# Table reads moved into the branches that use them, SyncE's three steps of a tile reordered, and a 64-byte shift of SBUF, in an attention and mixture-of-experts kernel

## The reference

```python
def _attn_ref(x, state):              # x [8,8,512,64], state [8,8,32,64]
    a = softmax(scale * x @ state.T);  xread = a @ state
    a2 = softmax(scale * state @ x.T); sread = a2 @ x
    return concatenate([xread, sread], axis=2)     # 4352 tokens of 512 columns

def _moe_ref(x, w_in, w_out):         # w_in [512,2048], w_out [2048,512]
    h = x @ w_in
    return (h * clip(h + 3, 0, 6) / 6) @ w_out

def _moe2_ref(x, w_gate, w_output_gate, w1, w2):   # 8 experts, w1 [8,512,1024], w2 [8,1024,512]
    e_idx = argmax(x @ w_gate, axis=1)             # each token goes to one expert
    for e in range(8):
        mask = e_idx == e
        out[mask] = gate_w[mask] * eom[mask, e] * (relu(x[mask] @ w1[e]) @ w2[e])
```

## Time and profile before

| | |
|---|---|
| three runs | 1202.80, 1205.89, 1206.66 us; median 1205.89 |
| profiled execution | 1207.43 us, of which the span, first to last instruction, is 1205.7 |
| TensorE | busy 1142.7 us (95%) |
| weight load | 893.1 us (74%), beside the matmuls |
| VectorE | busy 636.8 us (53%) |
| ScalarE | busy 463.8 us (38%) |
| GpSimd | busy 76.9 us (6%) |
| granted TensorE clock, mean | 0.975 of full |
| DMA | 131.65 MB, mean 109 GB/s |

### The profile page before, as it was taken

One profiled execution on the slowest core, in us unless ns is written; L12 is line 12 of the kernel. 1 busy time (PEld: TensorE's weight loads), 2 busy tenths in 40 slices (PEclk: granted clock), 3 DMA queues, 4 the chain that ended last, 5 costly groups with the idle time before them and its releaser, 6 DMA issues.

```text
span 1205.7 us, 21805 instructions
## 1 busy us (share of the span) xinstructions
PE 1142.7 (95%) x6358; PEld 893.1 (74%) x6359; DVE 636.8 (53%) x1247; ACT 463.8 (38%) x780; POOL 76.9 (6%) x96
## 2 busy tenths in 40 slices
PE   9999999999999999999999978889989999869996
PEld 7777777777777777777779866667868888657784
DVE  6675564646546456456644382554453444545543
ACT  4454443444344434444443422443332223333321
POOL 0000101001001010010100110000000000000001
PEclk9999999999999999999999989998989999979999
DMA  9111011101011010000200945747474544746442
GB/s 368 72 36 35 36 36 71 36 1 71 36 35 53 19 71 35 36 36 1 88 18 2 320 144 170 227 158 253 125 261 141 158 145 124 256 138 194 138 146 78
DMA packets 98819, 131.65 MB, mean 109 GB/s; under 512 B 13967, under 2 KB 75023, under 8 KB 94352
## 3 DMA queue, kind: packets, MB, share of 16 engines
q1 hardware_dynamic: 91360, 89.35, 23.4%
q10 hardware_dynamic: 1584, 23.07, 5.1%
q0 software_dynamic: 5760, 17.90, 4.1%
HBM read 85.86 MB, written 45.47 MB: 109 GB/s over the span
## 4 chain that ended last, share of the span: by engine, by line
PE 74%; ACTq 6%; issue 5%; DVE 5%; DMA 3%; ACT 3%; SPq 1%; DVEq 1%; POOL 0%; POOLq 0%
PE y_ps L853 32%; PE h_ps L835 15%; PE y_ps L926 9%; ACTq L442 5%; PE y_ps L910 5%; PE h_ps L910 5%; PE a_ps L810 2%; PE h_ps L825 2%; DMA hid_mv<-hidden 2%; DMA hidden<-expert_hid 1%; ACT we L1074 1%; DVE we L481 1%; DVE act_raw L1551 1%; ACT act_t_hi L1111 1%; PE a_ps L713 1%
## 5 line engine op out<-in xcount | busy, mean ns | idle before, releaser
L853 PE MATMUL y_ps<-w_out_hi,hid_hi 128*128 128x512 f32 x544 | 218.8, 402 | 0.0
L853 PE MATMUL y_ps<-w_out_hi,hid_lo 128*128 128x512 f32 x544 | 212.6, 391 | 0.0
L853 PE MATMUL y_ps<-w_out_lo,hid_hi 128*128 128x512 f32 x544 | 212.3, 390 | 0.0
L926 PE MATMUL y_ps<-we,act_t_hi 128*128 (+1 forms) x608 | 189.1, 392 | 5.4 <-DVE act_t_lo L1558 4.3
L835 PE MATMUL h_ps<-att_hi,mix 128*128 128x512 f32 x512 | 185.3, 405 | 0.1
L1364 DVE SCALAR_TENSOR_TENSOR hid<-hid,h_ps 128x512 f32<-128x512 f32 (+1 forms) x144 | 94.4, 655 | 169.9 <-ACT hid L1033 169.9
L1033 ACT ACTIVATE hid<-h_ps,three 128x512 f32<-128x512 f32 (+1 forms) x144 | 95.3, 662 | 179.1 <-PE h_ps L835 155.5
L853 PEld LDWEIGHTS y_ps<-w_out_hi,hid_hi 128*128 128x128 f32 x544 | 102.1, 188 | 50.6 <-issue 30.4
L926 PEld LDWEIGHTS y_ps<-we,act_t_hi 128*128 128x128 f32 x608 | 114.8, 189 | 31.2 <-issue 6.2
L1373 DVE TENSOR_TENSOR hid_lo<-hid,hid_hi 128x512 fp32r<-128x512 f32 (+1 forms) x144 | 94.8, 658 | 70.4 <-ACT hid_hi L1041 69.9
L910 PE MATMUL h_ps<-we,xg_t_hi 128*128 (+1 forms) x304 | 102.8, 421 | 28.3 <-DVE we L481 14.4
(11 more groups left out here) (216 smaller groups left out, 1457.7 us busy)
## 6 DMA issues: line engine op xcount, KB each, us to landing
raw<-in_w ACTq DMA_DIRECT2D x11, 2048.0 KB, 8.9
hidden<-expert_hid SPq DMA_DIRECT2D x76, 256.0 KB
hid_mv<-hidden SPq DMA_DIRECT2D x152, 128.0 KB, 2.9
xg<-buckets SPq DMA_DIRECT2D x164, 64.0 KB
xb<-in_x_rows SPq DMA_DIRECT2D x8, 1024.0 KB, 4.8
x_t<-in_x_t SPq DMA_DIRECT2D x7, 1024.0 KB, 4.8
buckets<-pad_row SPq DMA_DIRECT2D x8, 774.0 KB, 8.6
raw<-in_w SPq DMA_DIRECT2D x3, 2048.0 KB, 7.7
```

The costliest lines, as they stand in the source:

```text
L853: i = pe.matmul(y_ps[:, t, :], (hid_hi, hid_lo)[hp][:, hid_at(b, j), t * P:(t + 1) * P], w_out_s[wp][:, j, :], start=(j == 0 and m == 0), ...
L926: i = pe.matmul(y2_ps[:, slot % 2, :], act_t[hp][:, slot % 2, f, :], we[:, bass.ds(w_at + (wp * WPART + KD * F + f * DM), DM)], start=(f = ...
```

## The change

Five things are done.

1. ACT reads the two SPLIT numbers ahead of its wait for `hid2_ps`, and everything else inside the branches that use it. In a tile that neither splits nor loads it reads two numbers, not nine.
2. ACT loads the raw `w2` in the same branch and the same tile as the raw `w1`, behind the four pieces of its split of `w2`. It waits there for `w2_ready` of the expert just split, which DVE gives at the end of its own four pieces. Before, this load came one tile later.
3. DVE reads its two SPLIT numbers ahead of `turn_hidden`; before, one behind `hidden_lo` and one at the end.
4. SP writes the hidden values first, then loads rows and gates, then reads back.
5. `rows` takes 8320 bytes instead of 8256, so that all behind it moves by 64 bytes.

```diff
-    o += CH * ROW * 4
+    ROWS_SIZE = -(-CH * ROW * 4 // P) * P
+    o += ROWS_SIZE
...
-    raw1_at = 163840 + CH * ROW * 4 + 2048
+    raw1_at = 163840 + ROWS_SIZE + 2048
...
         def body(t):                                   # SP
-            if not (isinstance(t.n, int) and t.n + 3 >= MT):
-                load_rows(t.plus(3))
-            load_gate(t)
             place = t.slot % 2
...
                 sp.dma_start(hidden[place, :, h * BANK:h * BANK + BANK], expert_hid[:, h * BANK:h * BANK + BANK]
                              ).then_inc(sem("hid_written"), 16)
+            if not (isinstance(t.n, int) and t.n + 3 >= MT):
+                load_rows(t.plus(3))
+            load_gate(t)
             wait(sp, "hid_written", 16 * HALVES * (t.n + 1))
...
                 rows_hi(t.plus(1))                     # ACT
+            split1 = entry(act, t, T_SPLIT)
+            if not t.first:
+                split2 = entry(act, t.plus(-1), T_SPLIT)
             for h in range(HALVES):
                 wait(act, "hid2_ps", HALVES * t.n + h + 1)
...
-            if not (t.first or is_b(t.n, 1)):
-                before_it = t.plus(-2)
-                load = entry(act, before_it, T_LOAD)
-                with act.If(load > 0):
-                    load_w2(entry(act, before_it, T_NEXT, E - 1), entry(act, before_it, T_ORD, E - 3) + 2)
-            if not t.first:
-                before_it = t.plus(-1)
-                load = entry(act, before_it, T_LOAD)
-                with act.If(load > 0):
-                    load_w1(entry(act, before_it, T_NEXT, E - 1), entry(act, before_it, T_ORD, E - 3) + 2)
-                split = entry(act, before_it, T_SPLIT)
-                n = entry(act, before_it, T_ORD, E - 1) + 1
-                other = entry(act, before_it, T_OTHER, WSLOT)
-                first_tile = entry(act, before_it, T_FIRST, MT)
-                with act.If(split > 0):
+                with act.If(split2 > 0):
+                    n = entry(act, before_it, T_ORD, E - 1) + 1
+                    other = entry(act, before_it, T_OTHER, WSLOT)
+                    first_tile = entry(act, before_it, T_FIRST, MT)
+                    load = entry(act, before_it, T_LOAD)
+                    e = entry(act, before_it, T_NEXT, E - 1)
+                    with act.If(load > 0):
+                        load_w1(e, n + 1)
...
                     split_hi(1, n, other)
-            split = entry(act, t, T_SPLIT)
-            n = entry(act, t, T_ORD, E - 1) + 1
-            other = entry(act, t, T_OTHER, WSLOT)
-            with act.If(split > 0):
+                    with act.If(load > 0):
+                        load_w2(e, n + 1)
+            with act.If(split1 > 0):
+                n = entry(act, t, T_ORD, E - 1) + 1
+                other = entry(act, t, T_OTHER, WSLOT)
                 wait(act, "hid2_ps", HALVES * t.n)
                 split_hi(0, n, other)
```

More of the change, by code:

```diff
@@ L1138, in body @@
                 hidden_hi(t.plus(-1))
-            if is_b(t.n, 1):
-                load_w2(entry(act, Tile(0, MT), T_NEXT, E - 1), 1)
-            if not (t.first or is_b(t.n, 1)):
-                before_it = t.plus(-2)
-                load = entry(act, before_it, T_LOAD)
-                with act.If(load > 0):
-                    load_w2(entry(act, before_it, T_NEXT, E - 1), entry(act, before_it, T_ORD, E - 3) + 2)
-            if not t.first:
-                before_it = t.plus(-1)
-                load = entry(act, before_it, T_LOAD)
-                with act.If(load > 0):
-                    load_w1(entry(act, before_it, T_NEXT, E - 1), entry(act, before_it, T_ORD, E - 3) + 2)
-                split = entry(act, before_it, T_SPLIT)
-                n = entry(act, before_it, T_ORD, E - 1) + 1
-                other = entry(act, before_it, T_OTHER, WSLOT)
-                first_tile = entry(act, before_it, T_FIRST, MT)
-                with act.If(split > 0):
+                if is_b(t.n, 1):
+                    load_w2(entry(act, Tile(0, MT), T_NEXT, E - 1), 1)
+                before_it = t.plus(-1)
+                with act.If(split2 > 0):
[6 more added lines that the diff above has]
+                        load_w1(e, n + 1)
                     if not is_b(t.n, 1):
@@ L1568, in body @@
                 put_out(t.plus(-3))
+            split1 = entry(dve, t, T_SPLIT)
             if not t.first:
+                split2 = entry(dve, t.plus(-1), T_SPLIT)
                 turn_hidden(t.plus(-1))
@@ L1575, in body @@
                 before_it = t.plus(-1)
-                split = entry(dve, before_it, T_SPLIT)
-                with dve.If(split > 0):
+                with dve.If(split2 > 0):
                     split_lo(dve, 1, entry(dve, before_it, T_ORD, E - 1) + 1, entry(dve, before_it, T_OTHER, WSLOT),
                              signal="w2_ready")
-            split = entry(dve, t, T_SPLIT)
-            with dve.If(split > 0):
+            with dve.If(split1 > 0):
                 split_lo(dve, 0, entry(dve, t, T_ORD, E - 1) + 1, entry(dve, t, T_OTHER, WSLOT), signal="w1_ready")
```

## The result

| | before | after |
|---|---|---|
| median | 1205.41 us (4 runs) | 1170.62 us (1167.76 to 1174.89, 4 runs) |
| ratio | | 0.9717 [0.9677, 0.9757] |
| profiled execution, its span | 1207.43, 1205.7 us | 1167.76, 1166.0 us |
| TensorE busy | 1142.7 us | 1127.7 us |
| mean granted clock | 0.975 | 0.988 |

1170.6 us were measured where 1171 was forecast. The ratio of 0.9717 makes the gain 34 us, the difference of the medians 34.8. So the trace after shows some 3 us less loss than a usual run has, and a term that comes out better by that much in it is no finding.

What follows compares the result with a forecast made beforehand. ACT's table reads, which leave it behind TensorE at changes of experts, were taken to cause most stage-two losses. 1207.4 - 29.6 (waits and clock) - 4.9 (alignment) = 1172.9, or 1171.4 from the median: forecast 1171, range 1156 to 1187.

Steps and rivals of the forecast that it cites:

- The 9.9 us: ACT's round in a plain tile before the change, table reads included, 1.1 us less than TensorE's.
- first(1): First TensorE block of tile 1: 3.1 us of wait and 2.8 of clock hang on DVE's table building and stay.
- second(1), second(3), first(4), first(5): TensorE blocks of early tiles: tile 1's 4.3 us wait goes; waits of 5.5, 0.4 and 2.1 us remain, plus 2.5 clock.
- pairs at 7, 12, 25, 28, ahead of second(T): Tiles where two raw loads follow closely: the late readback delays TensorE's second block, 1.8 us each, 7 us in all.
- first(28): TensorE's first block of tile 28: late hidden values delay its weight split, 6.9 us of wait and 1.8 of clock remain.
- second(37), the end: Last tile's second block: today's 1.1 us wait stays and SP's order adds 1.1 us, 2.2 in all.
- alignment: Moving SBUF data by 64 bytes makes each tile's first TensorE block 0.13 us faster, 4.9 us in all; bounds +1 and -10.
- one block from E + 6.3 to E + 18.5: Both raw loads' packets flow unbroken, counted from E, the end of tile T's first TensorE block; readback through at E + 20.5.
- rival 1: Raw loads and SP's transfers don't collide, or whole packets hold: the pairs cost 0, 22 us lost or less, 1159; chance 0.20.
- the rule of whole packets: Queues: 9 to 17 descriptors a turn, so the readback passes within the first raw load; the sum 7 us better.
- SP's order is hidden in plain tiles: Plain tiles: readback at most 1.5 us later, landing at E + 10.4, hidden by 8.7 us.
- rival 2: Pairs of raw loads cost 5 us each, first(28) 14, and waits above 2 us bring half clock: 1189; chance 0.20.

Runs made afterwards that it cites:

- e2: The kernel before with only ACT's table reads changed, the second weight load still one tile later: 1181.76 us, 0.9787.
- e6: The kernel before with ACT's raw weight loads cut to a sixteenth, so that they don't hold up SP's transfers: 1197.52 us, 0.9913.
- e7: The changed kernel with ACT's raw weight loads cut to a sixteenth: 1159.61 us, 0.9601.
- e1: The kernel before with only the 64-byte shift of what lies behind `rows` in SBUF: 1204.77 us, 0.9978.
- e5: The kernel before with only SP's new order of writes, loads and readback: 1213.31 us, 1.0045.

## Why the prediction was right

**What bounded the kernel: right.** Nine reads made ACT's round nearly as long as TensorE's 11.07 us, and each change of experts left it behind. The 9.9 us that I worked out are rough: the row that they rest on ends in a wait for TensorE. Rounds without one take 9.4 us (copies of rows at 932.83 and 942.20), and one with a turn of the loop 12.5 (910.40 and 922.88), by the pause that I had nowhere. The mean over four tiles is 10.2, which leaves 0.9 us to spare and not 1.1. e2 takes only reads and gains 25.7 us; e6 takes only the transfers away, and the waits for rows stay. The plain tile came out as worked out: no idle time behind `act_t_hi`, and two reads that lie within the 8.3 us in which ScalarE waits for TensorE anyway.

**The ledger**, place by place, waits and clock in the profiled execution:

| place | forecast | measured |
|---|---|---|
| first(1) | 5.9 | 3.3 + 1.8 |
| second(1), second(3), first(4), first(5) | 8.0 + 2.5 clock | 0.3 + 1.5 + 0.8 + 3.0, clock in the rest |
| pairs at 7, 12, 25, 28, ahead of second(T) | 7 | 0 |
| first(9), by ACT | 0 | 2.1 |
| first(28) | 8.7 | 7.6 + 1.9 |
| second(37), the end | 2.2 | 2.6 |
| clock elsewhere, tiles 1 to 5 too | | 1.9 |
| sum | 34.3 | 26.8 |
| alignment | -4.9 | -1.7 ahead of stage two, -0.8 in it |

The sum of the savings, 34.5 us, met the medians' 34.8 by luck, because two terms that failed offset each other: the alignment brought 2.5 where I had 4.9, and the ledger then 34.8 - 2.5 = 32.3 where I had 29.6.

**The step "one block from E + 6.3 to E + 18.5" failed.** The two raw loads are 6.6 us apart as forecast (856.51 and 863.12 at tile 12), each a microsecond or two later than forecast, but their packets aren't one block. Around tile 12 SP's queue (q1) and ACT's (q10) moved, from 862 to 863 and from 863 to 864 us (packets, MB, share of 16 engines):

```profile
q10 hardware_dynamic: 29, 0.48, 113.8%
q1 hardware_dynamic: 30, 0.02, 6.1%
...
q1 hardware_dynamic: 409, 0.20, 68.5%
q10 hardware_dynamic: 17, 0.02, 4.7%
```

From 862 to 863, with the raw load flowing, both have the same number of packets, as in the earlier trace rows. But turns of one packet each are the best that SP gets: from 858 to 861 us, with the readback waiting, q1 moved one packet while q10 moved 67. From 863 to 864 us the first load has drained and the second hardly begun (0.02 MB), and in this gap q1 moves 409 packets, and 358 more in the microsecond behind it, in which q10 has 15: the rest of the readback, of whose 1024 packets 272 had gone ahead of the load. With E = 850.3 it was in by E + 15.8, when DVE began on it, not at E + 20.5. It took 8.2 us from issue to landing (the median of its four transfers; 2.7, 6.8 and 6.8 at tiles 7, 25 and 28); I had written that 9 or less would be rival 1. So rival 1 holds for the pairs, which cost nothing and not 7 us, by the gap and by the packets ahead of the load, both of which I had named as a bound, and not by the rule of whole packets: the Trainium skill's "DMA: Bandwidth & Descriptors", section Queues, rings and completion order (Arbitration), has 9 to 17 descriptors to a turn. The trace after has 49 packets of 16 KB against 48 of SP's from 861 to 863 us, one for one.

**first(28): right in size, 9.5 us against 8.7, and half right in mechanism**: a raw load does hold up tile 26's hidden values, but by another transfer and for a smaller part of the wait. I had tile 26's readback wait behind tile 25's. It was tile 26's *write* that the load held up. The chain there:

```profile
1004.54 0.34 ACTq L1125
...
1007.67 7.42 DMA hidden<-expert_hid
...
1017.06 2.86 DMA hid_mv<-hidden
1019.94 0.72 DVE act_raw L1552
...
1029.13 2.92 PE h_ps L912 x6
```

The load is issued at 1004.54; a write issued 3 us later takes 7.42 us to land, not 2.32; then the readback (2.86, undisturbed), `act_raw`, ACT, the split, and TensorE at 1029.13. `act_raw` begins at E + 25.9 where I had the readback landing at E + 27.8. e7 shows how this divides: 5.6 us would be there without any load, not 2.6, and 2 come from it, not 4.3. The term came out right by luck, with two parts that were wrong by 3.0 and 2.3 us in opposite directions.

**The SBUF part: the size failed, and its place.** -4.9 us was read off the difference of `first` and `second`; e1 measured -2.6, with `first` unchanged. The price was bounded by +1 and -10 for a reason, and the value taken from the wrong rows: stage one's L835, which I had named beside them, gave 1.8.

**"SP's order is hidden in plain tiles" holds only beside part 1.** In the changed kernel it is true. On the kernel before it costs 5.4 us, since nothing there has slack for it. The forecast never priced the part alone, and the expectation for e5, which did, had the wrong sign.

**Tiles 1 to 5 were better than forecast** by 3 or 4 us: the readback of tile 3, forecast 5.5 late by the block, was 1.5 late. It is the failed step once more. Nor do waits above 2 us always bring the half clock, as rival 2 has it: in the trace after, the blocks behind the waits of 3.04 us at first(5) and 2.05 at first(9) ran at full pace, 5.7 us each. That ACT would be late anywhere else I had excluded; it was at first(9), where `xg_t_hi` came at 809.75, behind 3.19 us of issue (reads, branches and a load) and an earlier wait for DVE.

Added up, the parts are: reads 25.7, alignment 2.6, and SP's order and the second load at about 4 each as seen from the changed kernel, neither clear of its interval, with DVE's reads at nothing that can be told. That makes 36 against 34.8 measured, but the parts depend on each other, as e5 shows, and needn't add up.

## What to carry to other kernels

When an engine's round is within a microsecond or two of the pace, count what its sequencer does that is not called busy: reads of a table in SBUF at half a microsecond each were worth 25.7 us here, all collisions with the raw loads 10.5 before and 11 to 14 after. Look at the turn of a loop by itself as well: here it held a pause of 2.7 us that stands in one tile of four only. The worth of an edit depends on who has slack: the same reordering of SP's stream cost 5.4 us while ACT was the bound and brought about 4 once it was not (the 4 are not clear of noise), so try such an edit in the kernel it is meant for. To see whether a transfer is held up, look at the queues microsecond by microsecond; a gap of a microsecond or two let through what six microseconds of the other's load had not.

## What was not expected of the hardware

- A transfer of 512-byte pieces beside one of 16 KB pieces gets at best a piece for a piece, 30 in a microsecond, and for three microseconds it got one against 67. As soon as the large one pauses it moves 409 pieces in a microsecond.
- Cutting the large one made things worse, by 14 to 18 us for four parts and 38 to 42 for eight. Each part costs ACT 0.5 us to issue, and pauses of 5.0 and 5.6 us follow at the turn of ACT's loop.
- Kernels that differ by a few instructions of ACT fall into two kinds. With 68 or more packets on the instruction queue ACT pauses 2.4 to 3.6 us at turns of its loop, with 32 or 33 it doesn't. The change moved the kernel from the first kind to the second, which the prediction did not foresee.
- Moving what lies behind `rows` by 64 bytes brought 2.6 us. It changed the mean of stage one's matmuls from 395 to 390 ns in a row neither of whose operands had moved, and from 404 to 402 in the row with a moved one, and left those of `first`, whose weights had moved, at 5.59 us for 24. Twenty-four matmuls of the other block take 5.46; neither alignment nor order explains it.
